# Attention scores as three fp32r products in place of one fp32 product, in a soft-MoE kernel on one core

## What is computed

```python
q_pool = q.reshape(B, H, S // 2, 2, D).mean(axis=3)
scores = scale * np.matmul(q_pool, k.transpose(0, 1, 3, 2))
scores = scores - np.max(scores, axis=-1, keepdims=True)
attn = np.exp(scores); attn = attn / (np.sum(attn, axis=-1, keepdims=True) + 1e-09)
attn_out = np.matmul(attn, v)
...
h = x @ w_in; g = np.where(h > 0, h, np.exp(np.minimum(h, 0)) - 1); x2 = g @ w_out
...
logits = x2 @ phi     # then softmax over tokens and over slots, 8 experts, and back to the tokens
```

## Time and profile before

| | |
|---|---|
| median of 3 runs | 945.69 us (945.55 to 945.79) |
| the profiled execution, its own time | 945.83 us |
| its span in the trace | 944.0 us |
| TensorE busy | 917.7 us, 97% |
| VectorE, ScalarE, GpSimd busy | 517.4, 394.1, 362.5 us |
| attention, heads 2 to 29 | from 47.34 to 427.95 us: 14 pairs of heads |
| dense stage begins | 462.27 us |

### The profile page before, as it was taken

The page is one execution under the profiler, slowest core; times in us unless marked ns, Lnnn a source line. Parts: engine busy times, 40 slices in busy tenths (PEclk is TensorE's granted clock), DMA queues, the critical chain, the costliest instruction groups (busy, mean ns, idle before and its releaser), DMA issues.

```text
span 944.0 us, 16864 instructions
## 1 busy us (share of the span) xinstructions
PE 917.7 (97%) x6544; PEld 703.3 (75%) x6544; DVE 517.4 (55%) x924; ACT 394.1 (42%) x740; POOL 362.5 (38%) x263
## 2 busy tenths in 40 slices
PE   5899999999999999999999999999999999999996
PEld 3566666666665666665799999999999999999833
DVE  6867766766676667665464433443443433533423
ACT  3555555655555556547442322322322322322302
POOL 1878888888888888888200000000000000000000
PEclk9999999999999999999999999999999999999998
DMA  6112112221220222202330000200000000267899
GB/s 237 45 58 77 42 60 76 77 76 52 76 76 27 76 77 76 94 1 71 100 121 1 1 2 1 90 1 1 1 1 1 1 1 1 90 225 227 283 384 331
DMA packets 47022, 76.33 MB, mean 81 GB/s; under 512 B 3296, under 2 KB 32608, under 8 KB 46944
## 3 DMA queue, kind: packets, MB, share of 16 engines
q1 hardware_dynamic: 46944, 75.26, 23.6%
HBM read 70.53 MB, written 4.72 MB: 80 GB/s over the span
## 4 chain that ended last, share of the span: by engine, by line
PE 49%; POOL 2%; SPq 1%; DMA 1%; issue 0%; ACT 0%; DVE 0%; POOLq 0%; ACTq 0%; DVEq 0%
PE psum L666 7%; PE psum L648 7%; PE psum L667 7%; PE psum L650 7%; PE psum L668 7%; PE psum L649 7%; POOL acc L1453 2%; PE psum L786 1%; SPq L464 1%; DMA ring<-in_w 1%; PE psum L704 1%; PE psum L686 1%; PE psum L710 1%; PE psum L597 0%; PE psum L691 0%
## 5 line engine op out<-in xcount | busy, mean ns | idle before, releaser
L1453 POOL TENSOR_TENSOR acc<-acc,pt 128x576 f32<-128x576 f32 x220 | 312.7, 1422 | 57.3 <-ACT pt L923 29.0
L923 ACT ACTIVATE pt<-psum 128x576 f32<-128x576 f32 x288 | 183.0, 651 | 129.7 <-PE psum L584 129.3
L583 PE MATMUL psum<-qs,kraw 64*128 64x288 f32 x576 | 183.2, 404 | 0.0
L584 PE MATMUL psum<-qs,kraw 64*128 64x288 f32 x576 | 183.2, 404 | 0.0
L1129 DVE TENSOR_REDUCE mx<-psum 128x1 f32<-128x512 f32 x256 | 162.3, 678 | 16.9 <-PE psum L528 15.3
L597 PE MATMUL psum<-pt,vs 128*64 128x288 f32 x1152 | 153.6, 412 | 0.0
L1302 DVE TENSOR_SCALAR gf<-gf 128x384 f32<-128x384 f32 x96 | 34.6, 360 | 195.6 <-ACT gf L1052 195.6
L666 PE MATMUL psum<-gh,W 128*128 128x384 f32 x384 | 133.5, 348 | 0.0
L1052 ACT ACTIVATE gf<-psum 128x384 f32<-128x384 f32 x96 | 47.2, 492 | 200.7 <-PE psum L650 200.1
L667 PE MATMUL psum<-gl,W 128*128 128x384 f32 x384 | 128.6, 335 | 0.0
L668 PE MATMUL psum<-gh,W 128*128 128x384 f32 x384 | 128.6, 335 | 0.0
(11 more groups left out here) (151 smaller groups left out, 1318.8 us busy)
## 6 DMA issues: line engine op xcount, KB each, us to landing
ring<-in_w SPq DMA_DIRECT2D x16, 1024.0 KB, 5.0
ring<-in_w SPq DMA_DIRECT2D x32, 512.0 KB, 7.9
qraw<-in_qT SPq DMA_DIRECT2D x16, 576.0 KB, 4.9
kraw<-in_kT SPq DMA_DIRECT2D x16, 576.0 KB, 3.7
vs<-in_v SPq DMA_DIRECT2D x16, 576.0 KB, 4.0
out<-ob SPq DMA_DIRECT2D x18, 256.0 KB, 3.3
wst<-in_w_in SPq DMA_DIRECT2D x16, 256.0 KB, 2.7
wst<-in_w_out SPq DMA_DIRECT2D x16, 256.0 KB, 2.9
```

Source lines behind the costliest of these rows:

```text
L583: mm(lo, kraw[0:64, p % NB, keys], qs[0:64, p % NB, q], start=False, stop=True).then_inc(s_Ta, 1)
L584: mm(hi, kraw[64:P, p % NB, keys], qs[64:P, p % NB, q], start=False, stop=True).then_inc(s_Tb, 1)
L923: act.activation(pt[:, i % NPT, :, :], t_pair(("T", h, kt))[:, :, 0:HALF], ACT.Exp, scale=SCALE)\
L1453: pool.tensor_tensor(a, first, pt[:, i % NPT, :, :], ALU.add).then_inc(s_acc, 1)
```

## The change

The score tile's plain fp32 product (two passes) becomes three fp32r products: khr x qhr, khr x qlr, klr x qhr, where `klr` = `kraw` - `khr` and `qlr` = `qs` - `qhr` are what rounding left. `khr` and `qhr` get three buffers (`NB`) and `qhr` all 576 queries. The remaining parts are made on VectorE: `keys_lo` in two halves of 576 columns, one in the odd head p (for pair p + 2) and one in the even head (for pair p + 1), each ahead of the late unit, and `queries_lo` behind the end unit of each even head from 2 on. For pairs 0 and 1 GpSimd makes them: pair 0 before its first add, pair 1 before the adds of head 1. To make room, `W_EARLY` goes from 6 to 5, so one weight tile's split moves into the dense stage.

```diff
-            mm(lo, kraw[0:64, p % NB, keys], qs[0:64, p % NB, q], start=False, stop=True).then_inc(s_Ta, 1)
-            mm(hi, kraw[64:P, p % NB, keys], qs[64:P, p % NB, q], start=False, stop=True).then_inc(s_Tb, 1)
+            n = p % NB
+            mm(lo, khr[0:64, n, keys], qhr[0:64, n, q], start=False, stop=False)
+            mm(hi, khr[64:P, n, keys], qhr[64:P, n, q], start=False, stop=False)
+            mm(lo, khr[0:64, n, keys], qlr[0:64, n, q], start=False, stop=False)
+            mm(hi, khr[64:P, n, keys], qlr[64:P, n, q], start=False, stop=False)
+            mm(lo, klr[0:64, n, keys], qhr[0:64, n, q], start=False, stop=True).then_inc(s_Ta, 1)
+            mm(hi, klr[64:P, n, keys], qhr[64:P, n, q], start=False, stop=True).then_inc(s_Tb, 1)
...
-    W_EARLY = 6
+    W_EARLY = 5
...
+        def keys_lo(p, part):
+            dve.wait_ge(s_khr, 2 * p + 2)
+            some = slice(part * (SK // 2), (part + 1) * (SK // 2))
+            dve.tensor_tensor(klr[:, p % NB, some], kraw[:, p % NB, some], khr[:, p % NB, some].bitcast(F32), ALU.subtract)\
+               .then_inc(s_klo, 1)
+
+        def queries_lo(p):
+            dve.wait_ge(s_qhr, p + 1)
+            dve.tensor_tensor(qlr[:, p % NB, :], qs[:, p % NB, :], qhr[:, p % NB, :].bitcast(F32), ALU.subtract)\
+               .then_inc(s_qlo, 1)
...
                 if kt == BLOCKS[1][0]:
+                    if h % 2 and p + 2 < NP:
+                        keys_lo(p + 2, 0)
+                    if h and h % 2 == 0 and p + 1 < NP:
+                        keys_lo(p + 1, 1)
                     reduce_items(s_items(h, LATE))
...
             reduce_items(s_items(h, END))
+            if h and h % 2 == 0 and p + 1 < NP:
+                queries_lo(p + 1)
             if h == 0:
                 queries(2)
...
         normalize(NH - 2)
-        weights_lo(W_EARLY - 1)
...
+        first_queries_lo(0)
+        first_keys_lo(0)
         for h in range(NH):
+            if h == 1:
+                first_keys_lo(1)
+                first_queries_lo(1)
...
-            act.copy(qhr[:, p % 2, 0:4 * P], qs[:, p % NB, 0:4 * P]).then_inc(s_qhr, 1)
+            act.copy(qhr[:, p % NB, :], qs[:, p % NB, :]).then_inc(s_qhr, 1)
```

More of the change, by code:

```diff
@@ L100, in soft_moe_kernel @@
         ("acc", [P, 2, 2, HALF], F32),
-        ("khr", [P, 2, SK], F32R),
-        ("qhr", [P, 2, SQ], F32R),
+        ("khr", [P, NB, SK], F32R),
+        ("qhr", [P, NB, SQ], F32R),
         ("bdq", [P, 2, P], F32R),
         ("onesel", [P, P], F32R),
-        ("rinv", [P, HALF], F32),
         ("nm2", [P, 2, 5, 65], F32),
         ("mx", [P, 2, 5, 2, 3], F32),
+        ("rinv", [P, HALF], F32),
         ("qraw", [P, 2, SQ], F32))
@@ L504, in ring_item @@
             p, u = item[1], item[2]
-            b = p % 2
+            b, n = p % 2, p % NB
             if u == 0:
@@ L514, in ring_item @@
             if u == NU - 1:
-                mm(lo[:, 0:REM], bdq[:, b, :], khr[:, b, 2 * KC:], start=True, stop=True).then_inc(s_Sf, 1)
+                mm(lo[:, 0:REM], bdq[:, b, :], khr[:, n, 2 * KC:], start=True, stop=True).then_inc(s_Sf, 1)
                 return
@@ L518, in ring_item @@
             if u == NU - 2:
-                mm(lo, bdq[:, b, :], khr[:, b, 0:KC], start=True, stop=True).then_inc(s_Sf, 1)
-                mm(hi, bdq[:, b, :], khr[:, b, KC:2 * KC], start=True, stop=True).then_inc(s_Sf, 1)
+                mm(lo, bdq[:, b, :], khr[:, n, 0:KC], start=True, stop=True).then_inc(s_Sf, 1)
+                mm(hi, bdq[:, b, :], khr[:, n, KC:2 * KC], start=True, stop=True).then_inc(s_Sf, 1)
                 return
@@ L527, in ring_item @@
             for to, queries, keys in pieces:
-                insA = mm(lo[:, to], qhr[0:64, b, queries], khr[0:64, b, keys], start=True, stop=True)
-                insB = mm(hi[:, to], qhr[64:P, b, queries], khr[64:P, b, keys], start=True, stop=True)
+                insA = mm(lo[:, to], qhr[0:64, n, queries], khr[0:64, n, keys], start=True, stop=True)
+                insB = mm(hi[:, to], qhr[64:P, n, queries], khr[64:P, n, keys], start=True, stop=True)
             insA.then_inc(s_Sa, 1)
@@ L573, in scores @@
                     pe.wait_ge(s_trc, 3 * p + 3)
-                pe.wait_ge(s_qs, p + 1)
-                pe.wait_ge(d_k[p % NB], 16 * (p // NB + 1))
+                if p < 2:
+                    pe.wait_ge(s_klo_first, 2 * p + 2)
+                    pe.wait_ge(s_qlo_first, p + 1)
+                else:
+                    pe.wait_ge(s_klo, 2 * (p - 2) + 2)
+                    pe.wait_ge(s_qlo, p - 1)
             if (h, kt) == (1, 0):
@@ L866, in keys_round @@
             act.wait_ge(d_k[p % NB], 16 * (p // NB + 1))
[L867 to L872, removed]
+            if p >= NB:
+                act.wait_ge(s_Ta, 18 * (p - NB + 1))
+                act.wait_ge(s_Tb, 18 * (p - NB + 1))
+            act.copy(khr[:, p % NB, 0:KC], kraw[:, p % NB, 0:KC]).then_inc(s_khr, 1)
+            act.copy(khr[:, p % NB, KC:SK], kraw[:, p % NB, KC:SK]).then_inc(s_khr, 1)
         def queries_round(p):
             act.wait_ge(s_qs, p + 1)
-            if p >= 2:
-                act.wait_ge(s_Sa, n_a[("S", p - 2, NU - 3)] + 1)
-                act.wait_ge(s_Sb, n_a[("S", p - 2, NU - 3)] + 1)
-            act.copy(qhr[:, p % 2, 0:4 * P], qs[:, p % NB, 0:4 * P]).then_inc(s_qhr, 1)
+            if p >= NB:
+                act.wait_ge(s_Ta, 18 * (p - NB + 1))
+                act.wait_ge(s_Tb, 18 * (p - NB + 1))
+            act.copy(qhr[:, p % NB, :], qs[:, p % NB, :]).then_inc(s_qhr, 1)
         def last_queries_round(p):
             b = p % 2
+            act.wait_ge(s_qhr, p + 1)
             if p >= 2:
@@ L978, in _ @@
                     weights_hi((2, 4, 8).index(kt))
-                if h == NH - 1 and kt in (2, 4, 8):
-                    weights_hi(3 + (2, 4, 8).index(kt))
+                if h == NH - 1 and kt in (2, 4):
+                    weights_hi(3 + (2, 4).index(kt))
             if h == 0:
@@ L1440, in _, with first_keys_lo, first_queries_lo @@
         pool.memset(onesel[64:65, :].bitcast(F32), 1.0).then_inc(s_sel, 1)
+        def first_keys_lo(p):
+            pool.wait_ge(s_khr, 2 * p + 2)
+            for part in range(2):
+                some = slice(part * (SK // 2), (part + 1) * (SK // 2))
+                pool.tensor_tensor(klr[:, p, some], kraw[:, p, some], khr[:, p, some].bitcast(F32), ALU.subtract)\
+                    .then_inc(s_klo_first, 1)
+        def first_queries_lo(p):
+            pool.wait_ge(s_qhr, p + 1)
+            pool.wait_ge(s_sel, 2)
+            pool.tensor_tensor(qlr[:, p, :], qs[:, p, :], qhr[:, p, :].bitcast(F32), ALU.subtract).then_inc(s_qlo_first, 1)
+        first_queries_lo(0)
+        first_keys_lo(0)
         for h in range(NH):
+            if h == 1:
+                first_keys_lo(1)
+                first_queries_lo(1)
             a = acc[:, h % 2, :, :]
```

11 lines of the change are left out of this document (7 added, 4 removed).

## The result

| | before | after |
|---|---|---|
| median (runs on the same chip) | 945.79 us (8 runs, 945.55 to 948.08) | 950.06 us (8 runs, 947.83 to 951.14) |
| ratio, 95% interval | | 1.0037 (1.0023 to 1.005) |
| profiled execution, and its span | 945.83, 944.0 us | 950.26, 948.4 us |
| sums of the last head begin | 455.33 | 456.49 |

The changed kernel is slower by 0.37% by this ratio (the two medians alone stand 0.45% apart). The time lies inside the range (936 to 955) and 3.2 us above the forecast of 946.9, which had put the time within 0.2% of before.

A forecast was written before the change was run, and what follows sets the result against it. TensorE was taken as always busy in attention, with every second tile in a block waiting for ScalarE's exponential. 945.83 + 1.8 (14 pairs) - 0.6 (first heads) = 947.0 profiled, 946.9 as median; range 936.0 to 955.0.

The forecast's parts named there:

- The tile: Score tile on TensorE: 0.615 us becomes 0.54, fp32r products 0.135 apart, a gain of 0.08 a tile.
- The third rival: fp32r products of 288 columns at 0.1225 each, the skill page's rule: a pair -0.23, 941.7 us; chance 0.10.
- fourth rival: Tiles bound by TensorE alone, VectorE hidden: -23 us, 922.7; chance 0.06.
- The blocks: Shorter tiles in a pair's score blocks: even head's first block -0.24, odd head's second block -0.16.
- tile 8: Odd head's second block: waits for tile 6's exponential, queued behind tile 5's, so only its own 0.08 is gained.
- `queries_lo` and u7: Subtraction outlasts GpSimd's add in flight, delaying u7 on TensorE; products with v +0.53, a pair +0.13.
- The first rival's case: `queries_lo` finds the port free and ends 0.73 earlier: a pair -0.60, 936.7 us; chance 0.22.
- `keys_lo`: Keys' subtractions lie in VectorE's idle time before u9 and u10, worst case 2.04: cost nothing.
- First heads -0.6: Heads 0 and 1, ordered by VectorE's reductions: a few shorter tiles give -0.6, between 0 and -1.5.
- the last heads: Last two heads: GpSimd's chain ends last, head 31's sums wait 1.10 for it, so shorter tiles give nothing.
- The sixth weight tile, 0: Its split moves to ScalarE and VectorE in the dense stage, covered by TensorE's products: 0, at most 1.2.
- The end: Program's end behind the dense stage: no term in the sum, so taken as unchanged.

The follow-up runs named there:

- the gain alone: Changed kernel with three fp32r products a tile, all of khr and qhr, and no subtraction of keys or queries on any engine: 934.37 us, ratio 0.987.
- e6: Changed kernel without VectorE's two keys_lo a pair, the third product using khr in place of klr: 948.87 us, ratio 1.0021.
- the second comparison: Changed kernel itself, run again unchanged, against the kernel before on the same chip: 950.24 against 947.13 us, ratio 1.0036.
- e7: Kernel before with 1152 already met waits more on TensorE in the dense stage, nothing else changed: 948.7 us, ratio 1.0018.

## Why the prediction was right and where it was wrong

**The tile: right.** An fp32r product of 288 columns takes 0.13, tile 5 to tile 7 1.58 (said: 1.59). The third rival, 0.1225 a product, is out (its own terms give 941.9, where 941.7 stands). The Trainium skill (TensorE: Matmul & The Clock Gate, section Part 1: The HAM clock gate) adds 2.5 ns to the columns' time; the trace disagrees for these products, with 10 ns or a little more (0.13 against 288 / 2.4 GHz = 0.120). That TensorE alone sets the time (fourth rival) would have given 922.7; the gain alone, with nothing in its way, stands at 934.37.

**The blocks: right in kind, too small.** I had -0.24 and -0.16, -0.40 in all, for the two blocks that make up the second part of a pair; they gave -0.52. In two pairs that I cut finer the odd head's second block gave -0.25 (said -0.16) and the even head's first -0.26 (said -0.24). The step that failed is tile 8 "behind the exponential of tile 6, which is queued behind tile 5's (0.63 apart)". The exponentials stand closer if the tiles do. ScalarE's row of after for those of the earlier trace rows:

```profile
55.72 1.19 ACT L935 ACTIVATE pt<-psum 128x576 f32<-128x576 f32 x2 [1.02 <-PE psum L596]
```

Two in 1.19 instead of 1.26: the second starts 0.55 behind the first, not 0.61 to 0.62. It was TensorE's pace that I had read as ScalarE's, and tile 8 gains its 0.08 too.

**`queries_lo` and u7: right.** 1.50 us (said 1.49), an idle time of 0.99 at u7 (said about 0.8), products with v 0.57 later behind u9 (said about 0.5), the pair +0.12 (said +0.13), or +0.11 by the medians of its parts. That the pair came out so close is luck: the second part gains 0.12 more than I had, the first loses 0.10 more, and the two errors cancel. The first rival's case, `queries_lo` alone, occurs in none of the 14 pairs of after: the shortest, 1.19, begins within an add too. It occurs in the first pair of e6.

**`keys_lo`: right.** 0.75 to 2.00 long, idle time left before u10 1.99 where it was 2.70, and nothing lost in 13 of 14 pairs (e6). In the first pair they cost some 0.5 us after all, by shifting GpSimd's adds against `queries_lo`, which the prediction hadn't considered.

**First heads -0.6: right.** u9 of pair 1 on TensorE stands at 54.17 instead of 54.78. In the last heads I had 0; from u9 of the last pair to the sums of head 31 it is 47.35 instead of 47.09, +0.26. **The sixth weight tile, 0: right**, 412.75 against 412.73 us.

**The end: wrong.** The step that failed is the sum itself, "945.83 + 1.8 - 0.6 = 947.0", in which the part behind the dense stage stands with nothing. I had asked of each engine what the change adds to it, and not what 1203 more instructions (18067 against 16864), 1152 of them TensorE's, do to a stage whose transfers are saturated and on the path. It was worth 3.26 us in the profiled execution, some 2 by the medians of the second comparison. Without it 950.26 would be 947.00, the sum to the digit, but luck has a part in that: the pairs' two errors are some 1.5 us each over 14 pairs and cancel. For the whole kernel the side was missed, and slower by over 0.2% had a chance of 0.33.

## What to carry to other kernels

When a faster product must be paid with extra vector work, look for where the vector engine idles and put the work there: the 13 pairs from 54 us on take 354.97 us with the 14 subtractions behind u5, 342.94 with them ahead of u9, and 341.75 with no subtraction at all, though each took longer ahead of u9 (1.96 against 1.50). A VectorE instruction with two inputs in SBUF next to a busy GpSimd is to be priced with the wait for the add in flight, or given a form with one input. And a change that adds instructions needs a term for stages it doesn't touch, if those are bound by transfers.

## What the runs showed of the hardware

Two inputs in SBUF against one: 1496 against 744 ns for 576 columns in the same place beside GpSimd's adds, and 752 with two inputs where no add was in flight at the start. Exponentials of 576 columns follow each other 0.55 us apart, less than one lasts (649 ns in the mean). 1152 waits that are already met, spread over TensorE's dense stage, cost that stage nothing: from the sums of head 31 to the last group but one of `d_tok` products it is 868.26 - 455.53 = 412.73 us in e7 and 868.08 - 455.33 = 412.75 before; but the end of the kernel, counted from that product on, was 1.4 us longer with them and 2.8 with twice as many, while the same waits on GpSimd left it at 75.92.
